# The order of the seven products of a Strassen-Winograd quad, each quad closed in itself

## The reference, cut to what matters

```python
x = attention(q, k, v, n_global, n_local)     # 2 x 768 tokens, 8 heads of 64: x is [1536, 512]
h = x @ w_in; g = h * sigmoid(h)              # [512, 2048], silu
x = g @ w_out                                 # [2048, 512]
logits = x @ w_gate                           # 8 experts
P = exp(logits - logits.max())
for _ in range(8):                            # Sinkhorn: rows, then columns
    P /= P.sum(1, keepdims=True) + 1e-09; P /= P.sum(0, keepdims=True) + 1e-09; P *= N / E
for e in range(8):
    out += P[:, e:e+1] * (np.maximum(x @ w1[e], 0.0) @ w2[e])   # [512, 1024], [1024, 512]
```

## Time and profile before

| | us |
|---|---|
| median of 3 runs | 1438.08 |
| range of the runs | 1435.07 to 1441.19 |
| profiled execution, its own time | 1440.61 |
| its span, first to last instruction | 1438.9 |
| PE busy | 1395.3 (97%) |
| DVE busy | 812.0 (56%) |
| ACT busy | 628.5 (44%) |
| POOL busy | 312.5 (22%) |
| mean granted TensorE clock | 0.988 of full |

### The profile page before, as it was taken

One profiled execution on the slowest core, in us unless ns is written; L12 is line 12 of the kernel. 1 busy time (PEld: TensorE's weight loads), 2 busy tenths in 40 slices (PEclk: granted clock), 3 DMA queues, 4 the chain that ended last, 5 costly groups with the idle time before them and its releaser, 6 DMA issues.

```text
span 1438.9 us, 20491 instructions
## 1 busy us (share of the span) xinstructions
PE 1395.3 (97%) x7345; PEld 1279.3 (89%) x7345; DVE 812.0 (56%) x1462; ACT 628.5 (44%) x1324; POOL 312.5 (22%) x381
## 2 busy tenths in 40 slices
PE   6998799999999999999999999999999999999998
PEld 5886799999999798998989889798998989899897
DVE  6554857674835764645546464665645546464552
ACT  5665625352514162533526254452534426253350
POOL 4121330312220302203021230402213030230200
PEclk9999999999988999999999999999999999999999
DMA  8310221221210212212122131222222121221201
GB/s 177 89 45 1 81 81 44 78 75 57 66 50 30 74 51 82 76 57 89 45 74 81 60 94 32 87 89 81 81 59 88 44 74 46 86 74 59 74 30 59
DMA packets 64783, 97.84 MB, mean 68 GB/s; under 512 B 18608, under 2 KB 33968, under 8 KB 64688
## 3 DMA queue, kind: packets, MB, share of 16 engines
q1 hardware_dynamic: 64688, 96.57, 22.6%
HBM read 93.41 MB, written 3.15 MB: 67 GB/s over the span
## 4 chain that ended last, share of the span: by engine, by line
PE 80%; DVE 6%; POOL 2%; ACT 1%; DMA 1%; issue 1%; ACTq 0%; DVEq 0%
PE a_ps L957 11%; PE a_ps L895 11%; PE b_ps L957 11%; PE c_ps L957 11%; PE b_ps L895 11%; PE c_ps L895 11%; PE d_ps L895 6%; DVE up_l L1188 2%; PE a_ps L954 1%; PE c_ps L954 1%; PE b_ps L954 1%; PE g_ps L976 1%; POOL up_raw L871 1%; DVE parts L1204 1%; PE d_ps L954 1%; DMA up_raw<-w_up 1%
## 5 line engine op out<-in xcount | busy, mean ns | idle before, releaser
L871 POOL TENSOR_TENSOR up_raw<-up_raw 128x256 f32<-128x256 f32 x78 | 77.6, 994 | 934.7 <-DMA up_raw<-w_up 934.7
L1188 DVE TENSOR_TENSOR up_l<-up_raw,up_h 128x512 fp32r<-128x512 f32 (+1 forms) x240 | 206.1, 892 | 51.8 <-ACT up_h L1021 51.6
L1021 ACT CAST up_h<-up_raw 128x512 fp32r<-128x512 f32 (+1 forms) x240 | 157.3, 686 | 89.1 <-POOL up_raw L876 76.2
L1057 ACT COPY b_ps<-a_ps 128x384 f32<-128x384 f32 x80 | 37.0, 463 | 306.4 <-PE a_ps L895 306.4
L1193 DVE TENSOR_TENSOR down_l<-down_raw,down_h 128x512 fp32r<-128x512 f32 x160 | 122.8, 775 | 28.2 <-ACT down_h L1031 28.1
L1031 ACT CAST down_h<-down_raw 128x512 fp32r<-128x512 f32 x160 | 98.5, 617 | 77.1 <-PE b_ps L957 65.5
L895 PE MATMUL a_ps<-xc_h,up_h 128*128 128x384 f32 x320 | 109.4, 342 | 6.9 <-DVE up_l L1188 6.9
L1234 DVE SCALAR_TENSOR_TENSOR hid_l<-parts,hid_h 128x384 fp32r<-128x384 f32 x128 | 76.1, 595 | 70.6 <-ACT hid_h L1089 68.5
L1089 ACT ACTIVATE hid_h<-parts 128x384 fp32r<-128x384 f32 x128 | 67.1, 524 | 100.2 <-DVE parts L1222 79.3
L895 PE MATMUL b_ps<-xc_h,up_h 128*128 128x384 f32 x320 | 107.5, 336 | 0.9 <-DVE up_l L1188 0.4
L895 PE MATMUL c_ps<-xc_h,up_h 128*128 128x384 f32 x320 | 107.9, 337 | 0.3 <-DVE up_l L1188 0.3
(11 more groups left out here) (190 smaller groups left out, 3445.4 us busy)
## 6 DMA issues: line engine op xcount, KB each, us to landing
up_raw<-w_up SPq DMA_DIRECT2D x80, 512.0 KB, 3.6
down_raw<-w_down SPq DMA_DIRECT2D x160, 256.0 KB, 2.7
q_sb<-qT SPq DMA_DIRECT2D x12, 256.0 KB, 3.4
k_sb<-kT SPq DMA_DIRECT2D x24, 128.0 KB, 3.6
v_sb<-v SPq DMA_DIRECT2D x24, 128.0 KB, 3.6
out<-x_sb SPq DMA_DIRECT2D x12, 256.0 KB, 2.6
vg_sb<-v SPq DMA_DIRECT2D x16, 4.0 KB, 1.7
nraw<-n_global SPq DMA_DIRECT2D x1, 1.0 KB, 2.6
```

Source lines behind the costliest of these rows:

```text
L871: nc.gpsimd.tensor_tensor(w[4], w[3], w[2], ALU.add).then_inc(up_summed, 1)
L1021: nc.scalar.copy(up_h[:, quad % UP_BUFS, lo:hi, :, :], up_raw[:, quad % RAWS, lo:hi, :, :]).then_inc(up_h_ready, 1)
L1057: nc.scalar.copy(b_ps[i % 2][:, 0:HALF], a_ps[i % 2][:, 0:HALF]).then_inc(kept, 1)
L1188: nc.vector.tensor_tensor(up_l[:, quad % UP_BUFS, lo:hi, :, :], up_raw[:, quad % RAWS, lo:hi, :, :], up_h[:, quad % UP_BUFS, lo:hi, :, :]. ...
```

## The change

The product order on PE becomes P1, P5, P6, P2, P7, P3, P4, all of the same quad. `made`, which numbers the products for the engines that wait, follows. P4 of a quad is no longer made in the next quad or in the down products. `add22` is now done before `add12`, on DVE and in the counts of `summed` (1 is `add22`, 2 is `add12`), and `hidden22` before `hidden12`. On ACT `keep_u3` comes before both, `hidden21` of the quad before stands directly behind `keep_p1`, and piece 2 of quad 3's weights is split between `hidden22` and `hidden12`. On DVE that piece stands last, behind `hidden12`.

```diff
             for quad in range(QUADS):
-                for name in ("P1", "P5", "P4", "P6", "P2", "P3", "P7"):
-                    if name != "P4":
-                        made[quad, name] = len(made) + 1
-                    elif quad % FP:
-                        made[quad - 1, name] = len(made) + 1
-                if quad % FP == FP - 1:
-                    made[quad, "P4"] = len(made) + 1
+                for name in ("P1", "P5", "P6", "P2", "P7", "P3", "P4"):
+                    made[quad, name] = len(made) + 1
...
 (PE, p5)
-                            pe.wait_ge(summed, 2 * (quad - 2) + 1)
+                            pe.wait_ge(summed, 2 * (quad - 2) + 2)
 (PE, others)
                         multiply(quad, "P2", a_ps[side], True)
...
+                        pe.wait_ge(kept, 4 * quad + 3)
+                        multiply(quad, "P7", b_ps[side], True)
                         pe.wait_ge(kept, 4 * quad + 2)
                         multiply(quad, "P3", c_ps[side], True)
-                        pe.wait_ge(kept, 4 * quad + 3)
-                        multiply(quad, "P7", b_ps[side], True)
+                        pe.wait_ge(kept, 4 * quad + 4)
+                        multiply(quad, "P4", d_ps, True)
 (PE, down)
-                            pe.wait_ge(hid_ready, 4 * (s * FP + f % FP) + (2 if f < FP else 4))
+                            pe.wait_ge(hid_ready, 4 * (s * FP + f % FP) + (3 if f < FP else 4))
...
-                                    if t == 3:
-                                        p4(quad3)
 (PE, main loop)
-                            if i > 0:
-                                p4(s * FP + i - 1)
 (ACT, quad_work)
                         if i > 0:
-                            hidden22(s, i - 1)
+                            hidden21(s, i - 1)
                         keep_p5(s, i)
...
-                        if i > 0:
-                            hidden21(s, i - 1)
...
-                        hidden12(s, i)
                         keep_u3(s, i)
+                        hidden22(s, i)
                         if i == 2:
                             split_up(quad + 1, 2)
+                        hidden12(s, i)
 (DVE, quad_work)
-                        if i > 0:
-                            hidden22(s, i - 1)
...
-                        add12(s, i)
+                        add22(s, i)
                         if s == 0 and i < 2:
                             for piece in range(len(PIECES)):
                                 split_up(quad + 1, piece)
+                        hidden22(s, i)
+                        add12(s, i)
                         hidden12(s, i)
-                        add22(s, i)
                         if i == 2:
                             split_up(quad + 1, 2)
 (ACT and DVE, down_work)
-                        hidden22(s, FP - 1)
+                        hidden21(s, FP - 1)
...
```

More of the change, by code:

```diff
@@ L914, in p5 @@
                         multiply(quad, "P5", c_ps[i % 2], False)
-                    def p4(quad):
-                        pe.wait_ge(kept, 4 * quad + 4)
-                        multiply(quad, "P4", d_ps, True)
                     def others(s, i, after):
@@ L935, in down @@
                         quad2, quad3 = s * FP + 2, s * FP + 3
-                        bank_free = [(hid_ready, 4 * quad2 + 1), (summed, 2 * quad2 + 1), (summed, 2 * quad2 + 2),
-                                     (hid_ready, 4 * quad3 + 1), (summed, 2 * quad3 + 1), (summed, 2 * quad3 + 2),
+                        bank_free = [(hid_ready, 4 * quad2 + 1), (summed, 2 * quad2 + 2), (summed, 2 * quad2 + 1),
+                                     (hid_ready, 4 * quad3 + 1), (summed, 2 * quad3 + 2), (summed, 2 * quad3 + 1),
                                      (hid_ready, 4 * quad3 + 1), (hid_ready, 4 * quad3 + 4)]
@@ L1053, in keep_p1 @@
                         if i >= 2:
-                            act.wait_ge(summed, 2 * (quad - 2) + 2)
+                            act.wait_ge(summed, 2 * (quad - 2) + 1)
                         elif s > 0:
@@ L1062, in keep_p5 @@
                         if quad > 0:
-                            act.wait_ge(summed, 2 * (quad - 1) + 2)
+                            act.wait_ge(summed, 2 * (quad - 1) + 1)
                         if i == 0 and s in turns:
@@ L1071, in keep_u2 @@
                         if quad > 0:
-                            act.wait_ge(summed, 2 * (quad - 1) + 1)
+                            act.wait_ge(summed, 2 * (quad - 1) + 2)
                         nc.scalar.copy(parts[:, U2, :], b_ps[i % 2][:, 0:HALF]).then_inc(kept, 1)
@@ L1101, in hidden12, with hidden22 @@
                     def hidden12(s, i):
+                        act.wait_ge(summed, 2 * (s * FP + i) + 2)
+                        hidden(s, i, 2, parts[:, C12, :], parts[:, C12, :], i, 1)
+                    def hidden22(s, i):
                         act.wait_ge(summed, 2 * (s * FP + i) + 1)
[L1103 to L1107, removed]
+                        hidden(s, i, 1, parts[:, C22, :], parts[:, C22, :], i + FP, 1)
                     def hidden21(s, i):
@@ L1146, in quad_work @@
                                 split_up(quad + 1, piece)
-                        hidden12(s, i)
                         keep_u3(s, i)
+                        hidden22(s, i)
                         if i == 2:
                             split_up(quad + 1, 2)
+                        hidden12(s, i)
                     def down_work(s):
-                        hidden22(s, FP - 1)
+                        hidden21(s, FP - 1)
                         split_up((s + 1) * FP, 0)
-                        hidden21(s, FP - 1)
                         turn = turns.index(s + 1) if s + 1 in turns else None
@@ L1244, in hidden12 @@
                     def hidden12(s, i):
-                        hidden(s, i, 1, parts[:, C12, :], parts[:, C12, :], i, 1)
+                        hidden(s, i, 2, parts[:, C12, :], parts[:, C12, :], i, 1)
                     def hidden22(s, i):
-                        hidden(s, i, 2, parts[:, C22, :], parts[:, C22, :], i + FP, 1)
+                        hidden(s, i, 1, parts[:, C22, :], parts[:, C22, :], i + FP, 1)
                     def hidden21(s, i):
```

## The result

The changed kernel takes 1460.25 us (median of 4, 1455.23 to 1462.06) against 1439.57 us of the kernel before in the same comparison (median of 4, 1435.07 to 1441.19): ratio 1.0143, 95% interval 1.0116 to 1.0170. That is 20.7 us slower. Forecast were 18.3.

What follows compares the result with a forecast made beforehand. PE's number of matmuls bounds the kernel and stays unchanged, so only late inputs matter: 12.2 relu, 7.1 silu, 1.0 step 0, -1.2 and -0.8 down stage sum to +18.3, 1456.4 us; 8 in 10 runs from 1446 to 1467.

Steps and rivals of the forecast that it cites:

- P6 of quad 3, relu: In relu steps P6 of quad 3 waits for piece 2 on DVE: 0.76 us in each of 16 steps, +12.2.
- P6 of quads 1 and 2, silu: In silu steps P6 of these quads comes late behind `keep_p1` on ACT: 0.65 us each.
- P6 of quad 3, silu: In silu steps P6 of quad 3 waits for piece 2 on DVE: 1.92 us, of which 0.38 was paid before.
- bank d given back, a silu step: Down products' wait at bank d for `hidden21` of quad 3 goes, as P4 comes three banks earlier: 0.45 us back.
- seams, a step: P4 leaves the down stage with two changes of bank group: about 0.06 us less a step, -1.2 over 20 steps.
- turn in step 11: Of the 1.9 us that the turn in a relu step costs, 0.8 is given back.
- step 0: Step 0, bound by weight splits in quads 0 to 2: between -2.1 and +2.4 us, taken as +1.0.
- gate's step: Taken as a relu step; could lose up to 3 us more, or its token sums wait up to 3.4 less.
- The covers cost nothing: Waits for `keep_p1`, `keep_u2` and `keep_u3`, now with one product beside each, fit by 0.14 us and cost nothing.
- rival 1: Thin covers of 0.14, 0.14 and 0.04 us break in nearly every quad at 0.05 each: +12, 1468 us; chance 0.09.
- The tail of the quad: DVE and ACT order at the quad's end puts piece 2 at 9.22, so P6 comes late; relu quads 1, 2 lose nothing.
- rival 2: Clock falls behind quad 3's stall, three products at half clock, 1.6 us a step: +31, 1487 us; chance 0.04.

Runs made afterwards that it cites:

- e1: Changed kernel, with piece 2 of quad 3's weights split ahead of `hidden12` on DVE: 1442.14 us, ratio 1.0028 to the kernel before.
- e8: Changed kernel, with piece 2 one place later still on DVE, behind `hidden21` of quad 2: 1481.5 us, ratio 1.0305 to the kernel before.
- e2: Changed kernel, with `keep_p1` of the next quad ahead of `hidden12` on ACT: 1464.63 us, ratio 1.0192 to the kernel before.
- e9: Changed kernel run once more, unchanged: one run, 1455.48 us.
- e3: Changed kernel, with piece 2 ahead of `hidden12` on DVE and next quad's `keep_p1` ahead of `hidden12` on ACT: 1436.41 us, ratio 0.9983 to the kernel before.
- e4: Kernel before, its product order kept, with piece 2 one place later on DVE, behind `hidden22` of quad 2: 1461.63 us, ratio 1.0160.

## Why the prediction was right, and where it was off

| term | forecast | measured | how |
|---|---|---|---|
| P6 of quad 3, relu | 0.76 | 0.80 | after; goes in e1, doubles in e8 |
| relu step in all, with the seams (the changes between quads and down banks) | 0.70 | 0.73 | step table |
| P6 of quads 1 and 2, silu | 0.65 | 0.66 | after; goes in e2 |
| P6 of quad 3, silu | 1.92 | 1.95 | after |
| bank d given back, a silu step | 0.45 | 0.20 | 0.73 before, 0.53 after |
| seams, a step | -0.06 | -0.07 | 61.90 in e1 against 61.97 |
| turn in step 11 | -0.8 | -0.45 | +0.28 against +0.73 |
| step 0 | +1.0 | +2.8, and -0.1 in e9 | the clock |
| gate's step | +0.7 | -0.4, and -3.5 in e9 | the clock, at three places |

The total came out within 2.4 us, and that is in part luck: the changed kernel's four runs span 7 us, and the terms of step 0 and of the gate's step, off by +1.8 and -1.1 in the profiled pair, partly cancel. The terms of the queues, which carry the forecast, are right one by one.

- *What bounds*: right. The time moved where an input of a product came late, and in step 0 and the gate's step where the clock fell; the added idle time is in the quads. All waits of PE behind the attention went from 17.8 to 33.8 us, +16 where about 18 were forecast.
- *The covers cost nothing*: right. With slack 0.14 and 0.04 no relu product but P6 of quad 3 was late. e3 overdrew one by 0.07 and paid 0.04, so rival 1 had about the price (0.05), but its premise, that covers of 0.14 and 0.04 break, was wrong.
- *The tail of the quad*: right in each instant. Piece 2 was forecast at 9.22 and stood there. e1, e2, e4 and e8 move one instruction each and get the forecast lateness to 0.1.
- *Bank d*: mis-sized, and by a term put at nothing. Of POOL's sums the forecast said only that nothing but `down_work` waits for them. But they run beside DVE. In the tail of quad 3 of a silu step (step 1 of the changed kernel, DVE and POOL) one subtraction takes 0.97 where 0.56 is usual:
```profile
253.05 0.97 DVE L1226 TENSOR_TENSOR hid_l<-parts,hid_h 128x384 fp32r<-128x384 f32 x1
```
```profile
252.82 0.79 POOL L869 TENSOR_TENSOR up_raw<-up_raw 128x256 f32<-128x256 f32 x1
253.69 0.93 POOL L871 TENSOR_TENSOR up_raw<-up_raw 128x256 f32<-128x256 f32 x1
```
All that leads to bank d stands behind it on the queues, and bank d came 0.42 late and cost 0.11 more (0.62 and 0.11 before, with one subtraction of 0.98 in the tail there too). Without the 0.41 the bank would have been on time; that is worked out, since no run keeps POOL away. What the runs do show: in e1 a second subtraction of the tail took 1.14 and 1.00 in steps 1 and 3, and bank d was 0.74 late there, 0.42 in step 2; step 3 of e9 is another such case (1.08, 0.74). The late P6 of quad 3 isn't the cause of the rest: it was 1.85 late in the changed kernel and 0.25 in e3, and bank d 0.42 late in both; in the old order it was 0.30 late before and 1.85 in e4, and bank d 0.62 in both.
- *Step 0*: mis-sized, and by rival 2, which I had priced at 1.6 in every step and which cost 2.8 in this one. Its P6 of quad 3 came 2.8 late and not 1.85, since POOL's sums ran beside DVE's work in quad 2 there (a split of 1.22 where 0.69 is usual, a subtraction of 0.98 where 0.56 is), and then three products took 0.9 longer each. e9 had the wait without the slow clock, and step 0 cost nothing. The reading against rival 2 was too coarse: a slice of the earlier trace rows is 36 us long and can't show a fall of 3 us. The kernel before had one in step 0 too, behind a wait of 4.7 us (length, busy PE, PEld, DVE, ACT, POOL, PEclk, DMA, GB/s):
```profile
154.00:157.00 3.00, 2.50 (x8) 2.50 (x9) 2.94 (x6) 0.68 (x3) 0.00 (x0) 0.59 0.45 108
```
- *Gate's step*: I took it as a relu step. In executions of kernels that treat it alike it lay between 87.8 and 91.6, so the -0.4 of one pair says nothing about the change. That it varies, and that the difference of the two executions of the changed kernel lies where the granted clock differs, is shown; why the clock falls in one and not in the other is open.
- The rule of the Trainium skill weighed above (TensorE: Matmul & The Clock Gate, "A second HAM failure mode: psum-queue depth-cycling"): by it the many short waits of the new order could have made the clock swing. The traces disagree for the waits of P6 in steps 1 to 3 and in the relu steps: behind all of them, up to 1.95 us, the products took 1.04, but for some 0.10 at the broken stream. The falls in e8 came behind single waits of 2.7, which is another thing than frequent short ones.

What the change itself is worth, once the tail is ordered for it: e3, 0.9983 of the kernel before, some 2 us. What repeats of it in the step lengths is small: 0.03 in a relu step (0.07 of seams less the 0.04 at P7) and 0.20 in a silu step, 1.3 in all with the turn. Step 0 and the gate's step are 1.3 and 1.6 shorter in e3's profile, but these two vary between executions of one kernel.

## What to carry to other kernels

When products are put into a new order, list for each the last instruction that must end before it, and place on each in-order queue by that list. Work for the next stage that used to stand ahead of a wait must stay ahead of it: one weight split of 0.69 us behind one wait was worth some 17 us here (ratio 1.0143 against 1.0028 in e1), and 23 in the old order. Read the slack in start-to-start times from the trace of before; a frame of a dozen such numbers gave the stalls of products in relu steps and silu steps 1 to 3 to about 0.1 us. It takes each instruction at its usual length, though: look also at what runs beside it, since POOL's sums made DVE instructions longer. And two kinds of step in one loop may want two orders.

## What the runs showed of the hardware

- The granted TensorE clock fell from 2.4 to 1.2 GHz behind some waits of 2.2 to 2.9 us and not behind others as long in the same kernel (0.50 and 1.00, 0.72 and 1.00 in the windows of the two executions above). Three products then cost 0.9 each more. This makes nearly all the difference between the two profiled executions of the changed kernel, 1462 and 1455, while every relu step repeats to 0.04. Of the four runs in the result only the slowest has a trace, but their mean clocks go the same way: 0.986, 0.988, 0.988 and 0.991 for 1462.1, 1461.0, 1459.5 and 1455.2 us.
- A DVE subtraction in fp32 took longer while POOL's additions of weights ran: 0.97 in place of 0.56 us for 384 elements, 1.22 in place of 0.69 for 512.
- A weight load freed by ACT came 0.51 to 0.56 behind the start of a 384-column copy, one freed by DVE 0.80 or 0.81 behind the start of a 512-element subtraction. A load freed 0.07 behind its turn cost 0.04; one freed well behind it cost its lateness and 0.07 to 0.14.
